# Turning TensorE's branch round and reordering the hand-over from attention to the first mixture-of-experts layer

## The reference

```
scores = where(keep, q @ k.T / 8 + bias, -1e9)
a = exp(scores - max) ; x = (a / (sum(a) + 1e-9)) @ v
P = exp(x @ w_gate - max)
for _ in range(8):
    P /= P.sum(1) + 1e-9 ; P /= P.sum(0) + 1e-9 ; P *= N / E
out = sum over e of P[:, e] * (relu(x @ w1[e]) @ w2[e])
second layer: rows assigned greedily by logit, 192 rows an expert, then relu(x @ w1[e]) @ w2[e]
```

## Time and profile before

| | before |
|---|---|
| median of 3 runs | 1431.8 us |
| the profiled execution | 1437.66 us |
| its span, first to last instruction | 1435.9 us |
| mean granted TensorE clock | 0.977 |
| TensorE busy | 1367.4 us, 95% |
| VectorE busy | 1012.7 us, 71% |
| ScalarE busy | 642.4 us, 45% |
| GpSimd busy | 95.8 us, 7% |

### The profile page before, as it was taken

How to read it: one execution, slowest core, us unless ns; L and a number is a source line. 1 busy time by engine, 2 the same in 40 slices (tenths; PEclk the granted TensorE clock), 3 DMA queues, 4 the chain that set the end, 5 groups by cost and what they waited for, 6 DMA issues and landing times.

```text
span 1435.9 us, 25226 instructions
## 1 busy us (share of the span) xinstructions
PE 1367.4 (95%) x9242; PEld 1236.9 (86%) x9242; DVE 1012.7 (71%) x2258; ACT 642.4 (45%) x1180; POOL 95.8 (7%) x112
## 2 busy tenths in 40 slices
PE   8996899999999999999999999999999956999997
PEld 5885889989998898998999899899899846888997
DVE  5566987787778888778777887877877557786000
ACT  5773445345445434544543553454455212343422
POOL 4550100000000000000000000000000000101111
PEclk9998899999999999999999999999999976999999
DMA  8751133313322332332233233133223005564430
GB/s 188 184 160 41 56 112 117 117 63 112 117 91 85 118 102 74 117 117 71 104 117 129 76 118 115 61 117 117 83 93 117 0 30 190 207 246 162 168 123 22
DMA packets 109489, 159.23 MB, mean 111 GB/s; under 512 B 37744, under 2 KB 43888, under 8 KB 109424
## 3 DMA queue, kind: packets, MB, share of 16 engines
q1 hardware_dynamic: 107376, 152.09, 32.1%
q0 software_dynamic: 2048, 6.29, 1.4%
HBM read 152.08 MB, written 6.29 MB: 110 GB/s over the span
## 4 chain that ended last, share of the span: by engine, by line
PE 85%; DVE 8%; ACT 2%; issue 2%; POOL 1%; DMA 1%; SPq 0%; another core or an unknown queue 0%; DVEq 0%; POOLq 0%; ACTq 0%
PE PS L1591 22%; PE PS L1592 22%; PE PS L1593 22%; PE PS L1747 5%; PE PS L1730 5%; PE PS L1556 2%; DVE G L1379 1%; PE PS L1527 1%; DVE w1lo L943 1%; PE PS L1777 1%; PE PS L1537 1%; PE PS L1694 1%; DVE w2lo L1078 1%; DVE xlo L949 1%; ACT sc L657 1%
## 5 line engine op out<-in xcount | busy, mean ns | idle before, releaser
L1591 PE MATMUL PS<-xhi,w1hi 128*128 128x256 f32 x1344 | 383.4, 285 | 11.4 <-DVE h_sum L1087 9.1
L1592 PE MATMUL PS<-xlo,w1hi 128*128 128x256 f32 x1344 | 382.8, 285 | 1.1 <-issue 1.1
L1593 PE MATMUL PS<-xhi,w1lo 128*128 128x256 f32 x1344 | 382.7, 285 | 0.0
L1591 PE MATMUL PS<-w2hi,hhi 128*128 128x512 f32 x768 | 299.5, 390 | 0.5 <-DVE w2lo L1078 0.5
L1592 PE MATMUL PS<-w2lo,hhi 128*128 128x512 f32 x768 | 299.3, 390 | 0.0
L1593 PE MATMUL PS<-w2hi,hlo 128*128 128x512 f32 x768 | 298.8, 389 | 0.0
L697 ACT COPY h_sum<-PS 128x512 f32<-128x512 f32 x144 | 84.6, 588 | 441.7 <-PE PS L1593 441.7
L1591 PEld LDWEIGHTS PS<-xhi,w1hi 128*128 128x128 f32 x1344 | 260.5, 194 | 14.2 <-issue 6.3
L1592 PEld LDWEIGHTS PS<-xlo,w1hi 128*128 128x128 f32 x1344 | 260.6, 194 | 1.8
L1593 PEld LDWEIGHTS PS<-xhi,w1lo 128*128 128x128 f32 x1344 | 260.4, 194 | 1.2 <-issue 1.2
L1105 DVE SCALAR_TENSOR_TENSOR acc<-PS,prob_e,acc 128x512 f32<-128x512 f32 x180 | 134.6, 748 | 78.2 <-PE PS L1593 78.2
(11 more groups left out here) (229 smaller groups left out, 1608.2 us busy)
## 6 DMA issues: line engine op xcount, KB each, us to landing
raw<-in_w SPq DMA_DIRECT2D x96, 1024.0 KB, 6.6
expert_weights<-in_w SPq DMA_DIRECT2D x10, 2048.0 KB, 13.7
raw<-in_w SPq DMA_DIRECT2D x6, 2048.0 KB, 7.9
vs<-in_v SPq DMA_DIRECT2D x16, 192.0 KB, 3.2
x_rows<-acc SPq DMA_DIRECT2D x3, 1024.0 KB, 8.2
vw<-in_v SPq DMA_DIRECT2D x16, 120.0 KB, 3.1
qs<-in_qT SPq DMA_DIRECT2D x4, 384.0 KB, 4.0
kp<-in_kT SPq DMA_DIRECT2D x4, 384.0 KB, 4.8
```

Of the source, the lines that this page charges most:

```text
L1591: T.matmul(o, whi, xh, start=first, stop=False, skip_group_check=shared)
L1592: T.matmul(o, whi, xl, start=False, stop=False, skip_group_check=shared)
L1593: return T.matmul(o, wlo, xh, start=False, stop=last, skip_group_check=shared)
```

## The change

Five things change, all before the steady loop of the dense mixture.

1. TensorE's branch is turned round: the wide version lies first in its code and the narrow one behind, so that the jump is taken at the start and none follows the narrow version. VectorE writes a second flag for it. Of the 24 + 12 spins there remain 8 before the branch, and 4 + 8 behind it. VectorE and ScalarE keep `path`.
2. ScalarE's wide version is written as nested loops over `hp` and `t`. It isn't run here, but it lies between the narrow version and what follows.
3. The 12 transposes of the last pair of heads come ahead of the 9 gate products of the first three quarters. They go to other banks, and ScalarE copies them behind the high part of w2, which it now makes first.
4. TensorE begins parts 0, 1 and 3 with the early half of x (k = 0) before the last x is there, and finishes them later. Part 0 is finished ahead of the transposes of the logits.
5. VectorE makes all low parts of x, the sums of w1 for unit 1 and the low parts of w2 ahead of the Sinkhorn rounds; they leave the list `first_unit`. ScalarE makes all high parts of x ahead of the logits' copy.

The diff, cut to its core:

```diff
         XT_DONE = H // 2 * NC
+        XT0_DONE = XT_DONE - NC + 1
         HT = QT // 2
         XBANK = [7, 6, 7]
-        XBANK_LAST = [0, 1, 2]
+        XBANK_LAST = [4, 5, 7]
+        BEGUN = [0, 1, 3]
         XT_STEP = {}
-        for pair_no in range(H // 2):
+        for pair_no in range(H // 2 - 1):
             for chunk in range(NC):
-                XT_STEP[2 * QT * (pair_no + 1) + (4 + 3 * chunk if pair_no < H // 2 - 1 else 4 + chunk)] = (pair_no, chunk)
+                XT_STEP[2 * QT * (pair_no + 1) + 4 + 3 * chunk] = (pair_no, chunk)
 
 
...
+        def path_wide_first(eng, attend):
+
+            eng.wait_ge(s_nar, 2)
+            is_wide = eng.value_load(narrow_i[0:1, 1:2], min_val=0, max_val=1)
+            with eng.If(is_wide):
+                attend(False)
+            with eng.Else():
+                attend(True)
+
         class Chain:
...
                 with act.Fori(0, H // 2) as i:
-                    for hp in range(2):
-                        for t in range(QT):
+                    with act.Fori(0, 2) as hp:
+                        with act.Fori(0, QT) as t:
                             for b in range(B):
-                                step(i * 2 + hp, hp, t, b)
+                                step(i * 2 + hp, t, b)
                     for c in range(NC):
                         x_copy(i, c)
...
                     x_hi(0, n, True)
+                w2_hi(0, 0)
+                x_hi(0, 0)
...
                     if STEPS - 6 <= s < STEPS - 6 + PARTS:
                         x_hi(0, s - (STEPS - 6), True)
                     if s in XT_STEP:
-                        i, c = XT_STEP[s]
-                        x_copy(i, c, XBANK_LAST if i == H // 2 - 1 else XBANK)
+                        x_copy(*XT_STEP[s])
+                w2_hi(0, 0)
+                x_copy(H // 2 - 1, 0, XBANK_LAST)
+                x_hi(0, 0)
+                x_copy(H // 2 - 1, 1, XBANK_LAST)
+                x_copy(H // 2 - 1, 2, XBANK_LAST)
+
+            def w2_hi(i, u):
+
+                act.wait_ge(s_raw2[u % 2], i * 16 + 16 * (u // 2 + 1))
+                if u:
+                    act.wait_ge(s_y, of_unit(i, TC, u - 1, 8))
+                act.copy(w2hi[:, u % 2], raw2[:, u % 2]).then_inc(s_w2h, 1)
...
-            x_hi(0, 0)
+            for n in range(1, PARTS):
+                x_hi(0, n)
             act.wait_ge(s_gg, 1)
             act.copy(group_rows[:], PS[0:GROUP * NC, GROUPS_BANK[0], :]).then_inc(s_ggc, 1)
-            for n in range(1, PARTS):
-                x_hi(0, n)
             part_copy(0, 0, 0, 1, 0)
+            part_copy(0, 0, 1, 2, 1)
...
             act.activation(shares, mk[:], ACT.Exp, bias=one1[:, 0:1], scale=1.0).then_inc(s_exp, 1)
 
-            part_copy(0, 0, 1, 2, 1)
             part_copy(0, 0, 2, 3, 0)
-            w2_hi(0, 0)
...
-            V.tensor_copy(narrow_i[:], narrow[:, 2:3]).then_inc(s_nar, 1)
+            V.tensor_copy(narrow_i[:, 0:1], narrow[:, 2:3]).then_inc(s_nar, 1)
+            V.tensor_scalar(narrow_i[:, 1:2], narrow[:, 2:3], 1.0, None, ALU.is_lt).then_inc(s_nar, 1)
...
                 ks = x_halves(c, early)
                 ins = V.tensor_tensor(xlo[:, n, ks], x_parts(c)[n][:, ks], xhi[:, n, ks].bitcast(F32), ALU.subtract)
-                if not early:
-                    ins.then_inc(s_xl, 1)
+                ins.then_inc(s_xl0 if early else s_xl, 1)
...
             def first_unit():
 
-                for n in range(SUMS):
-                    w1_sums(0, 1, n)
-                    yield
-                for k in range(FC):
-                    w2_lo(0, 0, k)
-                    yield
                 h_add(0, 0, 0)
...
 
             for n in range(SUMS):
                 x_sums(0, n)
-            x_lo(0, 0)
-            x_lo(0, 1)
+            for n in range(PARTS):
+                x_lo(0, n)
+            for n in range(SUMS):
+                w1_sums(0, 1, n)
             dve.wait_ge(s_lg, 1)
             dve.wait_ge(s_warm, 1)
             ch.step(V.tensor_copy(mk[:].rearrange("p (c j) e -> p c j e", c=NC), logit_groups[0]), "lg", SINK_AT)
             ch.step(V.tensor_reduce(one1[:, 0:1], mk[:].rearrange("p t e -> p (t e)"), AX.X, ALU.max), "rmax", SINK_AT)
-            x_lo(0, 2)
-            x_lo(0, 3)
+            w2_lo(0, 0, 0)
+            w2_lo(0, 0, 1)
             dve.wait_ge(s_par, 1)
             ch.step(V.tensor_scalar(one1[:, 0:1], one1[:, 1:2], -1.0, None, ALU.mult), "nmax", SINK_AT)
-            for n in range(4, PARTS):
-                x_lo(0, n)
+            w2_lo(0, 0, 2)
+            w2_lo(0, 0, 3)
             dve.wait_ge(s_exp, 1)
             aside = first_unit()
...
+            def part_block(n, f, k):
+                fs = slice(f * P, (f + 1) * P)
+                return three(PS[:, PART_BANK[n], f * HC:(f + 1) * HC], w1hi[:, n, k, fs], w1lo[:, n, k, fs],
+                             xhi[:, n, k, :], xlo[:, n, k, :], PART_OPENS[n] and f == 0 and k == 0, k == 1, True)
+
+            def begin_part(n):
+
+                pe.wait_ge(s_w1l, n + 1)
+                pe.wait_ge(s_xl0, n + 1)
+                for f in range(2):
+                    part_block(n, f, 0)
...
+                begun = x == 0 and n in BEGUN
+                if x == 0 and not begun:
+                    pe.wait_ge(s_xl0, n + 1)
+                for f in range(2):
+                    for k in range(begun, 2):
+                        ins = part_block(n, f, k)
+                ins.then_inc(s_pd, 1)
...
                 last = H // 2 - 1
-                pe.wait_ge(s_gate, 32)
+                begin_part(0)
+                begin_part(1)
                 pe.wait_ge(s_oh, last * NC + 2)
-                gate_products(0, range(DC - 1), x0)
                 pe.wait_ge(s_ev, 4 * last + 5)
                 for c in range(NC):
                     x_transposes_of(last % 2, c, XBANK_LAST)
-                pe.wait_ge(s_oh, XT_DONE + 2)
-                gate_products(0, [DC - 1], x0)
-
-            spin(24)
-            pe.wait_ge(s_q0, 2)
-            spin(12)
-            path(pe, lambda is_narrow: attend_window() if is_narrow else attend_full())
+                pe.wait_ge(s_gate, 32)
+                gate_products(0, range(DC - 1), x0)
+                begin_part(3)
+
+            spin(8)
+
+            def attend(is_narrow):
+                spin(4)
+                pe.wait_ge(s_q0, 2)
+                spin(8)
+                if is_narrow:
+                    attend_window()
+                else:
+                    attend_full()
+
+            path_wide_first(pe, attend)
+            pe.wait_ge(s_oh, XT_DONE + 2)
+            gate_products(0, [DC - 1], x0)
+            h_part(0, 0, 0, 0)
             logit_columns(0)
...
-            h_products(0, 0, 0)
+            for n in range(1, PARTS):
+                h_part(0, 0, n, 0)
```

69 lines of the change are left out of this document (31 added, 38 removed).

## The result

The changed kernel takes 1423.78 us (median of 6 runs, 1423.19 to 1427.97) against 1431.77 us of the kernel before on the same chip (6 runs, 1430.89 to 1432.79): a ratio of 0.9947 [0.9934, 0.996], 8.0 us faster. On two other chips it came to 0.9937 [0.991, 0.9964] and 0.9929 [0.9894, 0.9964]. Forecast were 10.2 us.

What follows compares the result with a forecast made beforehand. TensorE bounds the steady loop, VectorE's queue the stretch ahead of it. 12.5 us gained there, less 2.1 given back and 0.2 at the start, make 10.2: 1431.8 to 1421.6 us, range 1418.5 to 1426.

Steps and rivals of the forecast that it cites:

- the hand-over: Stretch from attention to the steady loop: 12.5 us gained by VectorE's queue, less 2.1 given back.
- the start: Spins and TensorE's turned jump before the first attention scores: costs 0.2 us, bounds 0 and 3.5.
- attention ends later by over 1 us: Sign at the end of attention that would show the prediction wrong; size over 1 us.
- ScalarE's jump: Ahead of ScalarE's high parts of x: jump over 43 rows, not 190, costs 0 us; bounds 0 and 4.99.
- VectorE's jump: Ahead of VectorE's sums of x: jump over 283 rows stays, costs 0 us; bounds 0 and 1.65.
- VectorE's queue: VectorE's work from 117.45 us before the loop: brings part 6 of unit 1 12.5 us earlier.
- The cross-check from the idle gaps: Before part 6 of unit 1: earlier start, VectorE's idle gaps and one Sinkhorn round add up to 12.1 us.
- the sum of pieces: VectorE's operations and rounds added up to part 6 of unit 1: 147.9 against 160.86 us, 12.9 us earlier.
- Given back: At part 6 of unit 2 TensorE waits about 2.1 us for VectorE; bounds 0 and 3.
- the start pays: Rival: late code behind TensorE's turned jump at the start costs 1.7 to 3.5 us, 1423.1 to 1424.9 us; chance 0.20.
- hidden under 4.82 us of waiting: Argument against the rival on the start: TensorE's equally long jump after 120 us lay under a 4.82 us wait.
- The slower case: Rival: the clock stays low in attention's first heads; 50 us of low clock cost 25, giving 1446 us; chance 0.05.

Runs made afterwards that it cites:

- e7: The kernel before with ScalarE's wide path in loops and nothing else of the change: 1440.26 us, ratio 0.9988.
- e5: The changed kernel run again as it is, on another chip: 1431.10 us, ratio 0.9937 to the kernel before.
- e9: The changed kernel run again as it is, on a third chip: 1430.88 us, ratio 0.9929 to the kernel before.
- e12: The kernel of e1 again, on one chip with the changed kernel of e9: 1428.86 us, ratio 0.989 to the kernel before.
- e1: The changed kernel with TensorE's branch and 24 + 12 spins as before, its jump behind attention: 1429.41 us, ratio 0.9934 to the kernel before.
- e11: The changed kernel with 2 + 4 spins behind TensorE's turned jump in place of 4 + 8: 1457.49 us.

## Why the prediction was right, and where it was off

The forecast was 1421.6 us; it came to 1423.78, inside the range. 8.0 us were gained where 10.2 were forecast; the hand-over came out as forecast, in part by luck, and the start did not. By its own sign, "attention ends later by over 1 us", the prediction was wrong there: attention ended 1.24, 2.62 and 1.56 us later.

- **ScalarE's jump.** Taken at 0 of 0 to 4.99 us. Right: no gap. But the reason why this counts was missed: e7 shows the term worth nothing while TensorE's own jump stays behind its last wait.
- **VectorE's jump.** Taken at 0; its sums of x have 0.21 us of idle time ahead, and start 0.3 us later than forecast once attention's shift is taken off (118.98 - 1.24 = 117.74 against 117.45). The row names ScalarE's first copy, but that had ended at 117.96, so the 0.21 us may be the jump's. In e5 the sums start at 117.47 with no idle time. The 1.65 us that the forecast had as its bound did not show.
- **VectorE's queue.** Forecast 12.5 us for part 6 of unit 1. It moved from 160.86 to 150.15, 10.71, and attention was 1.24 later: 11.95. The cross-check from the idle gaps (12.1) was nearer than the sum of pieces.
- **Given back.** Forecast 2.1 us, measured 1.57 in the changed kernel and 1.57 in e9 and e12. This error and the one above cancel, which is luck: forecast -10.4 for the hand-over, measured -10.15 to -10.45.
- **The start.** This is the term that was mis-sized: 0.2 us, measured 1.24 in the first trace and 1.56 and 2.62 in later ones. It is the rival "the start pays", with its 1423.1 to 1424.9 us. The step that failed is my argument against it, that TensorE had gone over a jump as long after 120 us "hidden under 4.82 us of waiting". The jump wasn't cheap there; uncovered, it takes 4.71 us itself (e7). A stall that lies under another was read as no stall. The row that tells, TensorE's packet of code at 121.9 us, lay 0.1 us ahead of the window of the earlier trace rows.
- **The Trainium skill's rule** (Runtime: NRT & Kernel Launch, section Instruction fetch mechanics: a jump beyond the pages held forces a fetch before anything goes on) holds for TensorE, by 4.40, 4.45, 4.53 and 4.71 us. It says less for the others. ScalarE's old jump, over 190 rows and so shorter than one page of 256, still cost 4.99 and 1.44 us; VectorE's, over 283, against which the forecast turned the rule, 0.21 at most. Which pages were held no trace shows, and the measured times decide. The fetch can be covered, too. In e1 and e12 the jump came with 24 products in TensorE's hands (2.7 us for the 18 of the gate, as from 118.06 to 120.76 above, and about 1 us for the six of part 3) and no wait between them and it, and 0.56 us or nothing was left of the stall. In the kernel before, the wait for ScalarE's third copy stood ahead of the jump, so little was in hand when it was taken, and the load of w1 was under way. The change moves the last gate products behind the branch; e1 says that this suffices, and that the turning adds nothing. The packets of code at 118.4 and 117.8 us, with products running until 120.5, show that the fetch runs beside them. How much of the gain is the cover and how much the early packet, ahead of the load, no run separates.
- **The slower case**, the low clock in attention, did not come with 20 spins, and came with 14 (e11). The forecast gave it 0.05; the margin is thinner than that suggests.

What stays open: whether a load that is moved shortens ScalarE's stall from 4.99 to 1.44 us, as the rows suggest, and why the low clock lasted 44 us in one execution and 171 in another with TensorE busy throughout. Nor is it shown what makes it come: not the number of spins alone, since 36 had it in ten of 100 executions, 20 behind a stall in none of 55, and 14 in six of 11.

## What to carry to other kernels

When an engine waits for another that stands still without a releaser, ask whether it has a stall of its own under that wait: removing one of two gains nothing, and a cheap-looking jump may be a covered one. Put a jump behind queued work and ahead of the next wait, and look whether a large load is under way when its code is fetched. And before a fill-in is cut or an idle engine is given work, look at what it shares with the busy one: the clock it keeps up, or the port it takes.

## What the hardware showed that I had not expected

- Two engines' stalls for code, ScalarE's of 4.99 us and TensorE's, 4.71 us when it stood alone, lay beside one another, with one named in the profile.
- In four stalls TensorE went on 2.7 to 3.1 us behind its packet of code, whether its DMA engines had been full or idle; what made a stall long was how late the packet came.
- Four GpSimd subtractions of 128x512 made VectorE's sums of 128x256 take 1.48 us in place of 0.42, and took 1.44 us each beside them, against VectorE's 0.60 undisturbed. The reduction behind them began 2.27 us after its input was ready, where the changed kernel's took 0.11.
- 20 spins in place of 36 gave no execution over 1450 us in 55, 14 gave six in 11; the clock can stay at 0.50 for 171 us of recorded full work.
